# Retention, MLP and gated attention on one core: states with full height, scaling of q and k on GpSimd, low parts moved, later means in two passes

## Chip, cores and metric

One core of a Trainium2 chip runs the whole program. The metric is the device time in microseconds. PE is TensorE (matmuls and transposes), DVE VectorE, ACT ScalarE, POOL GpSimd, SP the engine that issues most DMAs.

## What is computed

Three stages follow each other, in fp32, with B = 2, 8 heads, 768 positions, head size 64 and model size 512. The first is a retention with one decay per head:

```python
for t in range(S):
    state = gamma[None, :, None, None] * state + np.einsum('bhd,bhe->bhde', k[:, :, t], v[:, :, t])
    y[:, :, t] = scale * np.einsum('bhd,bhde->bhe', q[:, :, t], state)
```

The second is a layer norm and an MLP with a residual, on the heads' outputs side by side:

```python
mu = np.mean(x, axis=-1, keepdims=True)
var = np.mean((x - mu) ** 2, axis=-1, keepdims=True)
xn = (x - mu) / np.sqrt(var + 1e-06) * g_ln
x = x + np.maximum(xn @ w_ch1, 0.0) @ w_ch2
```

The third mixes four causal attention experts by a gate that keeps the best two. The change doesn't touch it.

## The kernel before

**Retention** works on 8 pairs of heads (`it` in the code, two heads side by side in 128 columns) and 6 chunks of 128 positions, in two groups `g` of three chunks. q and k are scaled by powers of the decay (`scale_rows`, line 289: four instructions of 128x384 for a pair, k and q for each group), turned by PE (`turn`, line 596) and evicted by ACT (line 933). Then follow for a group the scores of a chunk with itself (`scores_of`, line 609), DVE's product with the causal mask (`apply_causal`, line 1149), and the chunk's own part of the output (`chunk_outputs`, line 622). What earlier chunks contribute goes through states: PE forms the outer products of k and v of five chunks (`key_values`, line 652), in PSUM bank 6, for each head 64x64, the two heads one above the other; DVE sums them up over the chunks (`states`, line 1160 copies the first, line 1165 adds the others) into `state`, a 128x128 tile for each chunk with the two heads as blocks on its diagonal and zeros elsewhere, which GpSimd has set once. PE multiplies these with the turned q (`state_outputs`, line 631), and ACT evicts the outputs to `x` (line 939).

Each engine runs its instructions in the order in which the program lists them, so the order is that of the loops over `it` at the ends of PE's and DVE's parts. PE lists pair `it + 1`'s turns, scores and outer products among pair `it`'s outputs; DVE scales pair `it + 2` between its mask products and states. SP issues the loads of pairs in the order k, q, v, three buffers deep: the k and q loads of pair n wait until pair n - 3 is scaled, its v load until the outputs of pair n - 3 are done, and the loads of the first two MLP weight tiles stand behind the last of them.

**The MLP** works in three turns of 512 positions (256 of each batch). All products are made of three passes of a shorter type (fp32r): operands are split into a high part (a rounding copy) and a low part (the rest). GpSimd splits the weights (`split_w1`, lines 492 and 494; `split_w2`); ACT writes the high parts of activations and DVE the low parts. The first turn's means come while retention still runs: DVE adds up heads (`first_sum`, line 1226), PE multiplies the sum with a 128x128 matrix of 1/512 (`first_mean`, line 639, one for each batch), DVE centres (`first_centre`, line 1232), ACT scales (line 951) and DVE writes the low part (`first_lo`, line 1238). The later two turns do the same within the turn ahead of them, by steps `f` of 16: `add_heads` at steps 9 and 10, `next_mean` (line 719, one fp32 product of 512 columns) after step 12's products, `centre` at steps 13 and 14. A step is 12 products of the first matrix (`hidden`, line 702) and 12 of the second (`project`, line 711).

## Time and profile before

| | |
|---|---|
| median of 3 runs | 482.41 us (482.4 to 483.24) |
| the profiled execution's own time | 483.22 us |
| its span | 481.5 us, granted clock 0.992 |
| busy | PE 460.7 us (96%), DVE 285.8 (59%), ACT 148.6 (31%), POOL 134.8 (28%) |
| chain that ended last | PE 84%, DVE 8%, issue 3%, ACT 3%, POOL 1% |

The span is the time from the first instruction to the last in the trace; the execution's own time includes what lies around it. The granted clock is the share of TensorE's full speed. Retention takes the first 76 us, the MLP the time to 338 us, attention the rest. A row of an order of time gives the start and the duration of one instruction, or of several alike that follow each other, and in brackets how long its engine had been idle before and what ended that.

### The profile page before, as it was taken

The page shows a single profiled execution, that of the slowest core. Times are in us where ns is not written, and L with a number is a line of the kernel's source. Part 1 is how long each engine was busy: PE and PEld are TensorE (multiplying, and loading weights), DVE is VectorE, ACT ScalarE, POOL GpSimd, SP SyncE. Part 2 cuts the span into 40 slices and gives each one's busy share as a digit, 9 for nine tenths or more (in the row PEclk, how much of TensorE's full clock was granted, in tenths as well). Part 3 has the DMA queues.
Part 4 walks back from the last instruction along what each step waited for, and adds up shares of the span by engine and source line. Part 5 has one row for each costly group of instructions (what it writes and reads, how often), then busy time and mean ns, then how long its engine had stood idle before and what let it go on. Part 6 is the DMA issues. An engine that isn't in the chain of part 4 may idle for free.

```text
span 481.5 us, 7501 instructions
## 1 busy us (share of the span) xinstructions
PE 460.7 (96%) x2762; PEld 395.5 (82%) x2762; DVE 285.8 (59%) x660; ACT 148.6 (31%) x341; POOL 134.8 (28%) x167
## 2 busy tenths in 40 slices
PE   7799979999999999999999999999999899999896
PEld 6688867888888888888788888888998799998775
DVE  3789965147633547852262886142627888888833
ACT  2334422001100311001031001131425677777833
POOL 2000007899950000000002000000501477666720
PEclk9899989999999999999999999999999999999999
DMA  7977502444400000000003000000135354343024
GB/s 172 222 173 180 141 1 66 132 131 132 131 23 0 0 0 0 0 1 0 0 13 98 0 0 1 0 1 0 23 92 129 95 124 113 88 115 83 1 100 164
DMA packets 65792, 33.04 MB, mean 69 GB/s; under 512 B 47584, under 2 KB 61920, under 8 KB 65760
## 3 DMA queue, kind: packets, MB, share of 16 engines
q1 hardware_dynamic: 64960, 32.43, 26.0%
q8 instruction: 19, 0.31, 0.3%
q10 hardware_dynamic: 800, 0.20, 0.2%
q14 instruction: 13, 0.11, 0.1%
HBM read 20.03 MB, written 3.15 MB: 48 GB/s over the span
## 4 chain that ended last, share of the span: by engine, by line
PE 84%; DVE 8%; issue 3%; ACT 3%; POOL 1%; DMA 0%; POOLq 0%; ACTq 0%; DVEq 0%
PE ps L702 27%; PE ps L711 27%; PE ps L784 5%; PE ps L835 4%; PE ps L756 3%; PE ps L803 3%; PE ps L609 3%; PE ps L818 2%; PE ps L862 2%; PE ps L622 2%; PE ps L631 2%; DVE a L1432 2%; PE ps L596 1%; DVE state L1165 1%; DVE a_low_lo L1440 1%
## 5 line engine op out<-in xcount | busy, mean ns | idle before, releaser
L1278 DVE SCALAR_TENSOR_TENSOR h_t_lo<-ps,h_t_hi 128x512 fp32r<-128x512 f32 x48 | 33.2, 692 | 126.7 <-ACT h_t_hi L988 126.7
L988 ACT ACTIVATE h_t_hi<-ps 128x512 fp32r<-128x512 f32 x48 | 28.7, 598 | 218.9 <-PE ps L702 218.9
L702 PE MATMUL ps<-xn_t_hi,w_hi 128*128 128x512 f32 x192 | 75.6, 394 | 0.7 <-DVE xn_t_lo L1238 0.7
L702 PE MATMUL ps<-xn_t_hi,w_lo 128*128 128x512 f32 x192 | 74.8, 389 | 0.0
L702 PE MATMUL ps<-xn_t_lo,w_hi 128*128 128x512 f32 x192 | 74.7, 389 | 0.0
L711 PE MATMUL ps<-w_hi,h_t_lo 128*128 128x512 f32 x192 | 74.7, 389 | 0.0
L711 PE MATMUL ps<-w_hi,h_t_hi 128*128 128x512 f32 x192 | 74.7, 389 | 0.0
L711 PE MATMUL ps<-w_lo,h_t_hi 128*128 128x512 f32 x192 | 74.7, 389 | 0.0
L554 POOL TENSOR_SCALAR a<-a,inv_den,weight 128x768 f32<-128x768 f32 (+5 forms) x48 | 34.0, 716 | 50.8 <-DVE inv_den L1452 50.4
L702 PEld LDWEIGHTS ps<-xn_t_hi,w_hi 128*128 128x128 f32 x192 | 36.1, 188 | 9.1 <-POOL w_lo L494 0.9
L702 PEld LDWEIGHTS ps<-xn_t_lo,w_hi 128*128 128x128 f32 x192 | 36.1, 188 | 7.7 <-issue 0.5
L711 PEld LDWEIGHTS ps<-w_hi,h_t_lo 128*128 128x128 f32 x192 | 36.1, 188 | 7.5
L702 PEld LDWEIGHTS ps<-xn_t_hi,w_lo 128*128 128x128 f32 x192 | 36.0, 188 | 7.5
L711 PEld LDWEIGHTS ps<-w_hi,h_t_hi 128*128 128x128 f32 x192 | 36.0, 188 | 7.5
L711 PEld LDWEIGHTS ps<-w_lo,h_t_hi 128*128 128x128 f32 x192 | 36.0, 188 | 7.5
L1040 ACT ACTIVATE a<-a,neg_max 128x768 f32<-128x768 f32 (+5 forms) x48 | 32.3, 674 | 14.5 <-DVE neg_max L1432 14.5
L1265 DVE STREAM_TRANSPOSE rows<-x 32x512 f32<-32x512 f32 x48 | 33.7, 702 | 1.4
L517 POOL TENSOR_SCALAR w_vg_hi<-raw_vg 128x1040 fp32r<-128x1040 f32 x1 | 1.1, 1064 | 118.8 <-DMA raw_wo<-in_moe_wo 118.8
L492 POOL TENSOR_SCALAR w_hi<-raw_w 128x512 fp32r<-128x512 f32 x16 | 10.8, 675 | 68.0 <-DVE head_sum L1226 66.8
L1432 DVE CUSTOM_DVE_ANT_0 a<-ps,masked 128x768 f32<-128x768 f32 (+5 forms) x48 | 27.8, 617 | 1.0 <-PE ps L803 1.0
L818 PE MATMUL ps<-ident,a 128*128 128x128 f32 x168 | 23.6, 276 | 3.5 <-DVE a_low_lo L1440 2.4
L818 PEld LDWEIGHTS ps<-ident,a 128*128 128x128 f32 x168 | 18.6, 141 | 6.6 <-POOL a L554 5.0
(140 smaller groups left out, 886.0 us busy)
## 6 DMA issues: line engine op xcount, KB each, us to landing
raw_w<-in_moe_w_ch SPq DMA_DIRECT2D x32, 256.0 KB, 2.9
k_twice_hi<-pj_hi SPq DMA_DIRECT2D x32, 96.0 KB, 2.1
k_twice_lo<-pj_lo SPq DMA_DIRECT2D x32, 96.0 KB, 2.1
out_y<-out_sb SPq DMA_DIRECT2D x12, 256.0 KB, 2.0
raw_k<-in_k SPq DMA_DIRECT2D x7, 384.0 KB, 4.3
raw_q<-in_q SPq DMA_DIRECT2D x7, 384.0 KB, 4.9
raw_v<-in_v SPq DMA_DIRECT2D x7, 384.0 KB, 3.2
q_both<-pj_hi SPq DMA_DIRECT2D x16, 96.0 KB, 2.1
```

Of the source, the lines that this page charges most:

```text
L554: pool.tensor_scalar(a[:, g % AB, c0:c1], a[:, g % AB, c0:c1], inv_den[:, u:u + 1], weight[:, u, e:e + 1], ALU.mult, ALU.mult).then_inc(s_ ...
L609: mm = pe.matmul(s_bank()[:, j, c], k_t[rows, it % 2, G * g + c, :], q_t[rows, it % 2, G * g + c, :], start=True, stop=True)
L702: mm = pe.matmul(ps[:, f % 2, :], w1[a_][:, f, kk, :], xn_t[b_][:, kk, :], start=(kk == 0 and p_ == 0), stop=(kk == KT - 1 and p_ == 2))
L711: mm = pe.matmul(ps[:, 2 + tau, :], h_t[a_][:, f % 2, tau * P:(tau + 1) * P], w2[b_][:, f, :], start=(f == 0 and p_ == 0), stop=(f == NF - ...
L784: mm = pe.matmul(pj_bank(n), w_qk[a_][n // 4 % 2][:, kk, :], x2[b_][:, b, kk, half_cols(n)], start=(kk == 0 and p_ == 0), stop=(kk == KT - ...
L818: mm = pe.transpose(flat(4, 6, s0 + P)[:, s0:s0 + P], a[:, g % AB, s0:s0 + P], ident[:, :])
L835: mm = pe.matmul(z_bank(top)[:, skip:HALF], ev[:, b * NC + sc, e].rearrange("p h d -> p (h d)"), (a_top if top else a_low)[part][:, sc, sk ...
L988: act.activation(h_t["hi"][:, f % 2, :], ps[:, f % 2, :], ACT.Relu).then_inc(s_hhi, 1)
L1040: act.activation(a[:, g % AB, c0:c1], a[:, g % AB, c0:c1], ACT.Exp, bias=neg_max[:, 2 * (g % AB) + w:2 * (g % AB) + w + 1], scale=-1.0, ac ...
L1265: dve.transpose(rows[quad(a_), :, :, :, quad(d_)].rearrange("p b k u d -> p (b k) u d"), x[quad(d_), :, U * n:U * n + U, quad(a_)]).then_i ...
L1278: dve.scalar_tensor_tensor(h_t["lo"][:, f % 2, :], ps[:, f % 2, :], 0.0, f32(h_t["hi"][:, f % 2, :]), ALU.max, ALU.subtract).then_inc(s_hl ...
L1432: dve.tensor_tensor_reduce(a[:, g % AB, c0:c1], sc_bank(g, c1)[:, c0:c1], masked[:, NC - 1 - i:NC, :].rearrange("p c t -> p (c t)"), -1.0, ...
```

## The change

There are four edits.

1. *Outer products and states.* The outer products go to blocks on the diagonal of 128x128 tiles in PSUM (five tiles of 128 columns, in bank 6 and the start of bank 7), so that their off-diagonal blocks keep the zeros that DVE writes there once at the start (a new instruction, 128x640). A state step is then one instruction of 128x128 in place of two of 64x64: five for a pair in place of ten. GpSimd's clearing of `state` goes. The first means move to other columns of bank 7. The outer products of pair 0 stand ahead of the second scores of that pair, and wait for the zeros; those of pair 6 now wait until the first centring has read bank 7.
2. *Scaling.* DVE scales pairs 0 and 1 only; GpSimd scales pairs 2 to 7, ahead of its first weight splits, whose wait for the last sum of heads is dropped.
3. *Low parts.* The four low parts of the first batch (`first_lo(0, kk)`) move from DVE's last turn of the loop to after it, behind one more sum. `first_mean(0)` moves into the next pair, behind `state_outputs`.
4. *Later means.* `next_mean` is two fp32r passes over a high and a low part of the sum in place of one fp32 product. ACT writes the high part at step 11 and DVE the low part at step 12; the product comes after step 13 and `centre` at steps 14 and 15.

Its core as a diff:

```diff
-            return ps[:, 6, 0:(NC - 1) * D].rearrange("p (c e) -> p c e", c=NC - 1)
+            return ps[:, 6:8, :].rearrange("p a n -> p (a n)")[:, 0:(NC - 1) * P].rearrange("p (c e) -> p c e", c=NC - 1)
...
-            pool.memset(state[:, :, :, :], 0.0).then_inc(s_const, 1)
...
-            pool.wait_ge(s_acc, sums_before(1))
+            def scale_pair(n):
+
+                for g in range(2):
+                    for which in "kq":
+                        if n == 2 and g == 0:
+                            pool.wait_ge(s_scaled[which], 2 * n)
+                        if n == 2 and (g, which) == (0, "k"):
+                            pool.wait_ge(s_tab_rest, 16)
+                        if n >= RB and g == 0:
+                            pool.wait_ge(s_t, 4 * (n - RB) + 4)
+                            if which == "k":
+                                pool.wait_ge(s_kv, n - RB + 1)
+                        scale_rows(pool, n, which, g)
+
+            for n in range(2, NIT):
+                scale_pair(n)
             split_w1(0)
             split_w1(1)
...
+                else:
+                    pe.wait_ge(s_zeros, 1)
+                if it == HP + 2:
+                    pe.wait_ge(s_xc, KT)
...
+            key_values(0)
             for it in range(NIT - 1):
                 scores_of(it, 1)
-                if it == 0:
-                    key_values(0)
...
                 state_outputs(it, 0)
+                if it == HP + 1:
+                    first_mean(0)
...
-                if it == HP:
-                    first_mean(0)
...
-                pe.wait_ge(s_acc, (KT - 1) * i + sums_before(2))
-                pe.matmul(mean_bank(), mean_of[:, :], head_sum[:, :], start=True, stop=True).then_inc(s_mean, 1)
+                pe.wait_ge(s_sumlo, i + 1)
+                for part in ("hi", "lo"):
+                    mm = pe.matmul(mean_bank(), mean_of[:, :], sum_part[part][:, :], start=(part == "hi"), stop=(part == "lo"))
+                mm.then_inc(s_mean, 1)
...
+                    if f == 11 and not last:
+                        act.wait_ge(s_acc, sums_before(i + 2))
+                        act.activation(sum_part["hi"][:, :], head_sum[:, :], ACT.Copy).then_inc(s_sumhi, 1)
...
-                for j in range(2):
-                    half = slice(j * D, (j + 1) * D)
-                    dve.tensor_copy(state[half, it % 2, 0, half], kv_bank()[half, 0]).then_inc(s_st, 1)
+                dve.tensor_copy(state[:, it % 2, 0], kv_bank()[:, 0]).then_inc(s_st, 1)
                 for c in range(1, NC - 1):
-                    for j in range(2):
...
+                    dve.wait_ge(s_st, (NC - 1) * it + c)
+                    dve.tensor_tensor(state[:, it % 2, c], kv_bank()[:, c], state[:, it % 2, c - 1],
+                                      ALU.add).then_inc(s_st, 1)
...
+            dve.memset(kv_bank(), 0.0).then_inc(s_zeros, 1)
...
+                    if not last and f == 12:
+                        dve.wait_ge(s_sumhi, i + 1)
+                        dve.tensor_tensor(sum_part["lo"][:, :], head_sum[:, :], f32(sum_part["hi"][:, :]),
+                                          ALU.subtract).then_inc(s_sumlo, 1)
...
-                elif it < NIT - 2:
-                    for n in "kq":
-                        scale_next(it + 2, n, 0)
-                else:
+                if it == NIT - 2:
                     states(it + 1)
...
-                if it == HP + 2:
-                    for kk in range(KT):
-                        first_lo(0, kk)
                 apply_causal(it + 1, 0)
...
-                for n in "kq":
-                    scale_next(it + 2, n, 1)
             first_sum(1, HP - 2)
+            for kk in range(KT):
+                first_lo(0, kk)
             first_sum(1, HP - 1)
```

Where the instructions moved: the first place is PE at the start, from the turns of pair 0's second group on (x6 stands for three chunks and two heads). Before, and then with the change:

```order
L596 MATMUL ps<-ident,scaled_k 128x128 x3
L596 MATMUL ps<-ident,scaled_q 128x128 x3
L609 MATMUL ps<-q_t,k_t 128x128 x6
L652 MATMUL ps<-raw_v,scaled_k 64x64 x10
L622 MATMUL ps<-prob,raw_v 64x128 x6
L631 MATMUL ps<-q_t,state 128x128 x2
```

```order
L616 MATMUL ps<-ident,scaled_k 128x128 x3
L616 MATMUL ps<-ident,scaled_q 128x128 x3
L674 MATMUL ps<-raw_v,scaled_k 64x64 x10
L629 MATMUL ps<-q_t,k_t 128x128 x6
L642 MATMUL ps<-prob,raw_v 64x128 x6
L649 MATMUL ps<-q_t,state 128x128 x2
```

The ten outer products stand ahead of the second scores now, directly behind the turns.

The second place is DVE from the states of pair 6 to the end of the loop and the mask product behind it (`prob`), before and with the change:

```order
L1160 COPY state<-ps 64x64 x2
L1165 TENSOR_TENSOR state<-ps,state 64x64 x8
L289 TENSOR_TENSOR scaled_k<-raw_k,decay_sb 128x384
L289 TENSOR_TENSOR scaled_q<-raw_q,decay_sb 128x384
L1149 TENSOR_TENSOR prob<-ps,causal 128x768
L1160 COPY state<-ps 64x64 x2
L1165 TENSOR_TENSOR state<-ps,state 64x64 x8
L1222 TENSOR_TENSOR head_sum<-x 128x256
L1238 SCALAR_TENSOR_TENSOR xn_t_lo<-centred,g_col,xn_t_hi 128x256 x4
L1149 TENSOR_TENSOR prob<-ps,causal 128x768
L1226 TENSOR_TENSOR head_sum<-head_sum,x 128x256 x2
L1149 TENSOR_TENSOR prob<-ps,causal 128x768
```

```order
L1184 COPY state<-ps 128x128
L1187 TENSOR_TENSOR state<-ps,state 128x128 x4
L1175 TENSOR_TENSOR prob<-ps,causal 128x768
L1184 COPY state<-ps 128x128
L1187 TENSOR_TENSOR state<-ps,state 128x128 x4
L1234 TENSOR_TENSOR head_sum<-x 128x256
L1175 TENSOR_TENSOR prob<-ps,causal 128x768
L1238 TENSOR_TENSOR head_sum<-head_sum,x 128x256
L1250 SCALAR_TENSOR_TENSOR xn_t_lo<-centred,g_col,xn_t_hi 128x256 x4
L1238 TENSOR_TENSOR head_sum<-head_sum,x 128x256
L1175 TENSOR_TENSOR prob<-ps,causal 128x768
```

The scaling between the mask products is gone, a pair's states are five instructions, and the four low parts stand behind the mask product of pair 7's first group, between two sums.

The third place is POOL behind its constants, with the semaphores that each instruction waits for, before and with the change:

```order
L486 AFFINE_SELECT masked<-masked 128x128 [waits s_const]
L492 TENSOR_SCALAR w_hi<-raw_w 128x512 [waits s_w1raw0,s_acc]
L494 TENSOR_TENSOR w_lo<-raw_w,w_hi 128x512 [waits s_w1hi]
L492 TENSOR_SCALAR w_hi<-raw_w 128x512 [waits s_w1raw1]
L494 TENSOR_TENSOR w_lo<-raw_w,w_hi 128x512 [waits s_w1hi]
```

```order
L491 AFFINE_SELECT masked<-masked 128x128 [waits s_const]
L295 TENSOR_TENSOR scaled_k<-raw_k,decay_sb 128x384 [waits s_load_k2,s_tab_rest,s_scaled_k]
L295 TENSOR_TENSOR scaled_q<-raw_q,decay_sb 128x384 [waits s_load_q2,s_scaled_q]
L295 TENSOR_TENSOR scaled_k<-raw_k,decay_sb 128x384 [waits s_load_k2]
L295 TENSOR_TENSOR scaled_q<-raw_q,decay_sb 128x384 [waits s_load_q2]
L295 TENSOR_TENSOR scaled_k<-raw_k,decay_sb 128x384 [waits s_load_k0,s_kv,s_t]
```

Pair 2's four instructions wait for loads and for DVE's scaling of pair 1 alone; from pair 3 on the first of a pair also waits until PE has turned the pair three before it. 19 more follow in this pattern, then the weight splits, whose first no longer waits for `s_acc`.

## Rows read from the trace of the kernel before

**Rows 1.** Stages: from:to, us, busy PE PEld DVE ACT POOL, clock, DMA, GB/s.
```profile
14.00:21.00 7.00, 6.15 (x61) 4.81 (x61) 3.99 (x8) 2.46 (x5) 0.00 (x0) 0.76 0.93 210
57.00:76.00 19.00, 14.24 (x146) 11.86 (x146) 14.10 (x38) 6.23 (x15) 3.74 (x4) 0.91 0.06 16
76.00:338.00 262.00, 262.00 (x1154) 216.00 (x1153) 129.45 (x210) 38.83 (x66) 61.09 (x62) 1.00 0.11 32
```

**Rows 2.** TensorE in order of time, from 9 us: start us, us, line, [idle before <-releaser].
```profile
9.49 0.94 PE L609 MATMUL ps<-q_t,k_t 64*128 64x128 f32 x12 [0.64 <-ACT q_t L933]
13.83 0.71 PE L631 MATMUL ps<-q_t,state 128*128 128x128 f32 x4 [2.02 <-DVE state L1165]
22.44 0.94 PE L609 MATMUL ps<-q_t,k_t 64*128 64x128 f32 x12
```

**Rows 3.** Orders of time of TensorE, VectorE and GpSimd, 60 to 76 us.
```profile
60.68 0.80 PE L652 MATMUL ps<-raw_v,scaled_k 128*64 128x64 f32 x20 [0.61 <-DVE scaled_k L289]
67.42 1.55 PE L622 MATMUL ps<-prob,raw_v 128*64 128x128 f32 x12 [2.97 <-issue]
75.53 0.47 PE L702 MATMUL ps<-xn_t_hi,w_hi 128*128 128x512 f32 x1 [0.69 <-DVE xn_t_lo L1238]
...
64.66 1.67 DVE L1238 SCALAR_TENSOR_TENSOR xn_t_lo<-centred,g_col,xn_t_hi 128x256 fp32r<-128x256 f32 x4
73.91 1.48 DVE L1238 SCALAR_TENSOR_TENSOR xn_t_lo<-centred,g_col,xn_t_hi 128x256 fp32r<-128x256 f32 x1 [0.25 <-ACT xn_t_hi L951]
...
73.84 1.26 POOL L494 TENSOR_TENSOR w_lo<-raw_w,w_hi 128x512 fp32r<-128x512 f32 x1
```

**Rows 4.** SyncE's issues in order of time; landing of raw_v (6.5 us) and of raw_q.
```profile
4.93 2.08 SPq L439 DMA_DIRECT2D raw_v<-in_v  x4
8.28 0.73 SPq L403 DMA_DIRECT2D raw_q<-in_q  x1
12.43 1.28 SPq L403 DMA_DIRECT2D raw_q<-in_q  x1
...
raw_v<-in_v SPq DMA_DIRECT2D x2, 96.0 KB, 2.3
...
DMA to landing us min/median/max: 2.2/4.7/6.5
```

**Rows 5.** VectorE in order of time, 11 to 16 us.
```profile
11.28 0.48 DVE L1160 COPY state<-ps 64x64 f32<-64x64 f32 x2 [2.12 <-PE ps L652]
13.81 0.96 DVE L1149 TENSOR_TENSOR prob<-ps,causal 128x768 f32<-128x768 f32 x1
14.68 0.55 DVE L289 TENSOR_TENSOR scaled_k<-raw_k,decay_sb 128x384 f32<-128x384 f32 x1
15.15 0.55 DVE L289 TENSOR_TENSOR scaled_q<-raw_q,decay_sb 128x384 f32<-128x384 f32 x1
```

**Rows 6.** Groups of VectorE and GpSimd by shape; line 1278: ns min/median/max, first and last start.
```profile
L1165 DVE TENSOR_TENSOR state<-ps,state 64x64 f32<-64x64 f32 x64 | 14.2, 222 | 2.0
...
L569 POOL TENSOR_TENSOR z_t_lo<-z_sum,z_t_hi 64x384 fp32r<-64x384 f32 x14 | 14.2, 1016 | 1.2
...
L1278 DVE SCALAR_TENSOR_TENSOR h_t_lo<-ps,h_t_hi x48: 691/692/693, 79.2 to 334.0; 128x512 fp32r<-128x512 f32 x48
```

**Rows 7.** TensorE in order of time, 40 to 59 us.
```profile
40.29 0.94 PE L609 MATMUL ps<-q_t,k_t 64*128 64x128 f32 x12 [0.26 <-ACT k_t L933]
51.57 0.94 PE L609 MATMUL ps<-q_t,k_t 64*128 64x128 f32 x12
58.32 0.94 PE L609 MATMUL ps<-q_t,k_t 64*128 64x128 f32 x12
```

**Rows 8.** Chain of waits, 141 to 150 us: start us, us, what.
```profile
143.85 0.86 PE ps L719 x2
144.72 2.77 PE ps L702 x12
147.48 2.72 PE ps L711 x12
```

More of the change, by code:

```diff
@@ L123, in retention_moe_program @@
             z_sum = sb(late, "z_sum", [P, 2, HALF])
+        with ExitStack() as early:
+            sum_part = {part: sb(early, f"sum_{part}", [P, N], F32R) for part in ("hi", "lo")}
         with ExitStack() as early:
@@ L268, in mean_bank, with first_mean_bank @@
             return ps[:, 7, :]
+        def first_mean_bank():
+            return ps[:, 7, P:P + U * P]
         def kv_bank():
[L271 removed]
+            return ps[:, 6:8, :].rearrange("p a n -> p (a n)")[:, 0:(NC - 1) * P].rearrange("p (c e) -> p c e", c=NC - 1)
         def part_of(g):
@@ L635, in first_mean @@
             def first_mean(b):
-                pe.wait_ge(s_const, 6)
+                pe.wait_ge(s_const, 5)
                 pe.wait_ge(s_acc, (HP - 1) * (b + 1))
-                pe.matmul(half_of(mean_bank(), b), mean_of[:, :], half_of(head_sum, b), start=True, stop=True,
+                pe.matmul(first_mean_bank(), f32(mean_of[:, :]), half_of(head_sum, b), start=True, stop=True,
                           skip_group_check=True).then_inc(s_mean, 1)
@@ L651, in key_values @@
                         rows = slice(j * D, (j + 1) * D)
-                        mm = pe.matmul(kv_bank()[rows, c], scaled["k"][:, it % RB, c, rows], raw["v"][:, it % RB, j, c],
+                        mm = pe.matmul(kv_bank()[rows, c, rows], scaled["k"][:, it % RB, c, rows], raw["v"][:, it % RB, j, c],
                                        start=True, stop=True)
@@ L727, in mlp @@
                     project(i, f - 1)
-                    if not last and f == 12:
+                    if not last and f == 13:
                         next_mean(i)
@@ L1157, in states @@
                     dve.wait_ge(s_y, y_turn(it - 2, 1) + 1)
-                for j in range(2):
-                    half = slice(j * D, (j + 1) * D)
-                    dve.tensor_copy(state[half, it % 2, 0, half], kv_bank()[half, 0]).then_inc(s_st, 1)
+                dve.tensor_copy(state[:, it % 2, 0], kv_bank()[:, 0]).then_inc(s_st, 1)
                 for c in range(1, NC - 1):
-                    for j in range(2):
-                        half = slice(j * D, (j + 1) * D)
-                        dve.wait_ge(s_st, 2 * (NC - 1) * it + 2 * c + j - 1)
-                        dve.tensor_tensor(state[half, it % 2, c, half], kv_bank()[half, c], state[half, it % 2, c - 1, half],
-                                          ALU.add).then_inc(s_st, 1)
-            def scale_next(n, which, g):
-                if n >= NIT:
-                    return
-                if n >= RB:
-                    dve.wait_ge(s_t, 4 * (n - RB) + 4)
-                    if which == "k":
-                        dve.wait_ge(s_kv, n - RB + 1)
-                scale_rows(dve, n, which, g)
+                    dve.wait_ge(s_st, (NC - 1) * it + c)
+                    dve.tensor_tensor(state[:, it % 2, c], kv_bank()[:, c], state[:, it % 2, c - 1],
+                                      ALU.add).then_inc(s_st, 1)
+            dve.memset(kv_bank(), 0.0).then_inc(s_zeros, 1)
             dve.wait_ge(s_tab, 16)
@@ L1307, in mlp @@
                             add_heads(i + 1, kk)
-                    if not last and f in (13, 14):
-                        centre(i + 1, 2 * (f - 13))
-                        centre(i + 1, 2 * (f - 13) + 1)
+                    if not last and f in (14, 15):
+                        centre(i + 1, 2 * (f - 14))
+                        centre(i + 1, 2 * (f - 14) + 1)
                     if last and f == 12:
```

23 lines of the change are left out of this document (9 added, 14 removed).

## Prediction

> **What bounds the kernel now.** I read the busy shares first: TensorE (PE) is busy 96% of the span, so a gain has to come from PE's idle time, from its clock, or from work that PE no longer does. The stage table tells where it idles: from 76 us on PE hardly waits, while in the first 76 us there are holes, and two stretches with a granted clock under 1 (full speed): a mean of 0.76 over 14 to 21 us and 0.91 over 57 to 76 us [rows 1]. The clock has two levels, 1.2 and 2.4 GHz, so these means are 3.4 us each at the lower level, and work at half speed loses half of that time, 1.7 us each. Before the first stretch PE had idled 2.02 us for the states [rows 2], before the second 2.97 us [rows 3]. I then read VectorE (DVE) in order of time against PE's waits: in the first 76 us DVE ends the long ones, directly or because what PE needs stands in DVE's queue behind other work.
>
> **Part 1, the start (states, and the outer products ahead).** PE is free at 8.85 us (9.49 less 0.64 of idle) and waits there for an eviction [rows 2]. The outer products of pair 0 move into this gap. They need the four v loads, issued in 2.08 us from 4.93 on, the last near 6.5; with 2.3 us to landing [rows 4] they are there at 8.8. So I start them at 8.85 and end them 0.80 later (a block of 20 has 0.80 in [rows 3]), at 9.65. States now take 2.53 us from 11.28 to 13.81 [rows 5]: ten instructions. Afterwards there are five of double width and height. No row shows that shape: 64 columns take 222 ns [rows 6], 384 columns 0.55 us [rows 5], so 1.03 ns for each further column and 288 ns for 128 of them; bounds are 222 and 550 ns. I take 0.29, near the narrow row, plus the 0.03 us by which the ten instructions are apart: 1.6 us, to 11.25. The mask product (0.87 to the next start, [rows 5]) ends at 12.1, and pair 1's scaling starts at 12.15 instead of 14.68. Its second instruction meets another limit: q of pair 1 is issued at 8.28 and lands a median 4.7 us later [rows 4], at 13.0, so it runs at 13.0 instead of 15.15: 2.15 us earlier, not 2.5, and PE's turns follow. The state wait of 2.02 shrinks to almost nothing and the remaining idle time is in pieces of 0.75 us or less, so I take the clock to stay at 2.4 GHz, which gives back 1.7 us. GpSimd's first pair, pair 2, waits for q of pair 2, issued at 12.43 and so there at 17.1 [rows 4]; its first q half is scaled at 18.2. PE wants it some 0.4 us ahead of its next scores (22.44 before, [rows 2], and about 18.6 after), just then; I take off 0.25 for that. **Start: 2.15 + 1.7 - 0.25 = 3.6 us.**
>
> **Part 2, scaling on GpSimd.** 24 instructions leave DVE, 4 for a pair. On GpSimd a two-input instruction with 384 elements per partition takes 1016 ns [rows 6], so a pair costs it 4.1 us. Its bounds are 0.55 (DVE's own row) and, were the broadcast operand to cost double, 2.03 us. PE's period is 6.75 us (51.57 to 58.32, a stretch without a wait, [rows 7]), so GpSimd has room up to 1.69 us for one. GpSimd idles in this stage now, and its input is early: SP issues pair n's k and q behind the v load of pair n - 1, which waits for the outputs of pair n - 4; PE turns pair n nearly two periods, 13 us, after those, and issue and landing take some 6 us of that. SP's queue keeps its order; its waits on scaled rows end no later than its wait on the outputs ahead of them. DVE keeps two mask products, five state instructions and a sum per pair: 1.74 + 1.6 + 0.35 = 3.7 us of 6.75, so the mask product comes as soon as the scores are there. Now it is late: at 40.29 PE waits 0.26 us [rows 7]; the view names an ACT copy, but the same instruction also waits on the mask product of the other half. From 22.44 to 58.32 are 35.88 us [rows 2, 7]; five periods of 6.75 and one mean product, for which I put half of the 0.86 us that twice the columns take [rows 8], make 34.18. **Middle: 1.7 us.** Moving that mean product later in the program keeps its cost; its four readers on DVE hold bank 7, for which PE's next outer products now wait, but PE has turns, scores and the outputs of half a pair to do in between.
>
> **Part 3, the end of the loop.** DVE computes the four low parts (1.67 us) from 64.66 on, ahead of the mask product of pair 7, and PE idles 2.97 us until 67.42; the outer products of pair 7 wait 0.61 us for DVE's scaling [rows 3]. Both go: the scaling is long done and the low parts move behind the mask product, into a gap in which DVE waits for an output. Next late is that mask product itself, behind states (1.6) and a sum: about 0.3 us. The half-speed stretch, 1.7 us, goes with the idle time ahead of it. Last, the 0.69 us of PE before the first hidden product [rows 3]: there one low part takes 1.48 us, where four took 1.67, and a GpSimd two-input instruction runs over the same time (73.84, 1.26 us). The change drops the wait that held GpSimd's first weight splits until this moment; they now run as soon as their load has landed, which SP issues behind the last v load, over 10 us earlier; so 0.69 goes too. **End: 2.97 + 0.61 + 1.7 + 0.69 - 0.3 = 5.7 us.** The Trainium skill's page "SBUF — State Buffer", section "Who interferes with whom", says that a DVE instruction with two SBUF inputs and a GpSimd instruction that reads SBUF exclude each other for the whole instruction, while one with a single SBUF input is free of it. The trace agrees: the low part with two SBUF inputs was held, and the 48 low parts that read PSUM took 691 to 693 ns all through GpSimd's splits [rows 6]. By the rule the loop's sums (two SBUF inputs) can be held by GpSimd's scaling, at most 1.02 us each; without the rule nothing is held. DVE's free 3 us a pair cover that either way.
>
> **Part 4, later means.** A mean product now takes 0.86 us, and the block after it 2.77 instead of 2.72 us [rows 8]: 0.91. The two passes are of the type of the hidden products, 12 in 2.72 us [rows 8], so 0.45 for two. Executed twice: **0.9 us.** The added eviction and subtraction (128x512 each, some 0.69 us as the low part of that width, [rows 6]) lie on ACT and DVE, which in this stage are busy 38.83 and 129.45 us of 262 [rows 1]. Centring moves one step later; the first normalised tile is then ready some 3 us after the last hidden product, and PE has 5.44 us of projections (24 products, twice the 2.72 of 12) until it needs it: nothing.
>
> **Sum.** 3.6 + 1.7 + 5.7 + 0.9 = 11.9 us. The profiled execution took 483.22 us, so it would take 471.3; it lies 0.8 over the median of the runs, 482.41, so the median becomes **470.5 us**.
>
> **Rivals.**
> A: *the clock still falls at the start, or loads set the pace there.* Half the 3.6 us hangs on the clock and two landings fit to within 0.1 or 0.2 us. Without the clock 1.7 us are missing, with loads or the held low part besides another 1 to 2: 472.2 to 474.5. For it speaks that by the reckoning above waits of 0.4 to 0.75 us stay close together near 12 to 15 us; against it that the long one is gone.
> B: *PE waits for GpSimd in each pair.* GpSimd's instruction is 0.47 us longer than DVE's; if all 24 were on the path, 11.2 us would come back: 481.7, the same as before. Against it: loads lie ahead by most of a period. The Trainium skill's "GPSIMD Engine Reference", section 4.1, advises against it: two-input elementwise work is to stay on VectorE, GpSimd being about half as fast. The trace agrees on the ratio (1016 ns against 0.55 us), but not that it must be paid.
> C: *slower.* GpSimd is the bound. Should the broadcast factors with three strides cost much more than the row of [rows 6], its four instructions set the period. Above 1.69 us each it costs time, above 2.2 it decides: 6 pairs x (4 x 2.2 - 6.75) = 12.3 us, all of the gain. At 2.5 us a pair takes 10: 470.5 + 19.5 = 490. Against it: the two GpSimd rows shown, 1016 ns for 384 elements and 1.26 us for 512 [rows 3, 6], agree on some 2.5 ns an element, and neither is near three times that.
>
> **How the numbers follow.** Forecast 0.66; A 0.23; B 0.03; C 0.04; better by 2 us or more (idle time I did not see as such) 0.04. The range takes the forecast with its bounds and A: 467.8 to 474.5. About 0.2%, 1 us, is what a measurement can tell here: B counts as the same with 0.02, C as slower with 0.04, the rest is faster, 0.94.
>
> **What would show it.** Right: PE's rows of scores with a period of 6.75 us and no wait above 0.3 us from the third pair on; granted clock 1.00 in all of the first 70 us; five state rows near 0.29 us a pair; GpSimd rows of 1.0 us; the first hidden product near 64.5 us (75.53 less 11.0); no low part above 0.5 us in front of it; mean products of 0.45 us. Wrong: a stretch of clock 0.5 after 12 us (A), turns that wait for GpSimd (B), GpSimd busy without a break through the loop (C), or a hidden product that waits at a step's turn, which would mean that the later centring isn't free.

## The result, and the profile after

The changed kernel takes **470.99 us** (median of 4 runs, 470.56 to 471.55) against 482.44 us before (482.4 to 483.24): a ratio of 0.9759, 95% interval 0.9743 to 0.9776. The forecast was 470.5 us, range 467.8 to 474.5. The profiled execution took 470.56 us, with a span of 468.8 us and a granted clock of 1.0.

The stages first, as in [rows 1]; retention now ends near 65 us, so the limits differ. Columns: from:to, us, busy PE PEld DVE ACT POOL, clock, DMA, GB/s.

```profile
14.00:21.00 7.00, 6.88 (x89) 5.80 (x90) 3.67 (x8) 2.73 (x6) 3.23 (x4) 1.00 1.05 238
57.00:65.00 8.00, 7.22 (x81) 5.83 (x78) 6.66 (x16) 2.73 (x6) 0.00 (x0) 1.00 0.01 2
65.00:326.00 261.00, 261.00 (x1153) 216.16 (x1152) 130.64 (x211) 39.85 (x68) 61.02 (x62) 1.00 0.12 33
```

Both stretches that had a clock of 0.76 and 0.91 have 1.00, that is 2.4 GHz all through. TensorE in order of time shows three marks that [rows 2, 3, 7] have too: the second half of pair 1's scores (18.92, was 22.44), that of pair 6's (53.09, was 58.32) and the first hidden product (64.34, was 75.53), and every wait of 0.3 us or more from 9 us to there.

```profile
9.01 0.80 PE L674 MATMUL ps<-raw_v,scaled_k 128*64 128x64 f32 x20 [0.61 <-issue]
12.83 0.55 PE L616 MATMUL ps<-ident,scaled_k 128*128 128x128 f32 x3 [0.62 <-DVE scaled_k L295]
18.92 0.94 PE L629 MATMUL ps<-q_t,k_t 64*128 64x128 f32 x12
53.09 0.94 PE L629 MATMUL ps<-q_t,k_t 64*128 64x128 f32 x12
58.68 0.88 PE L642 MATMUL ps<-prob,raw_v 128*64 128x128 f32 x12 [0.30 <-issue]
62.84 0.88 PE L642 MATMUL ps<-prob,raw_v 128*64 128x128 f32 x12 [0.48 <-issue]
64.34 0.47 PE L723 MATMUL ps<-xn_t_hi,w_hi 128*128 128x512 f32 x1
```

Between the marks lie what the prediction called start, middle and end. Of the waits of [rows 2, 3], those of 2.02, 0.61 and 0.69 us are gone, and 0.30 is left of that of 2.97.

VectorE's groups by shape up to 65 us, and after them GpSimd's (line, engine, operation, count | busy us, mean ns | idle before):

```profile
L1187 DVE TENSOR_TENSOR state<-ps,state 128x128 f32<-128x128 f32 x32 | 9.3, 291 | 1.1
L1250 DVE SCALAR_TENSOR_TENSOR xn_t_lo<-centred,g_col,xn_t_hi 128x256 fp32r<-128x256 f32 x6 | 2.6, 479 | 0.2 <-ACT xn_t_hi L974 0.2
L1184 DVE COPY state<-ps 128x128 f32<-128x128 f32 x8 | 2.3, 291 | 4.1 <-PE ps L674 4.1
...
L295 POOL TENSOR_TENSOR scaled_q<-raw_q,decay_sb 128x384 f32<-128x384 f32 x12 | 10.1, 840 | 4.5 <-DMA raw_q<-in_q 3.6 <-PE ps L616 0.9
L499 POOL TENSOR_TENSOR w_lo<-raw_w,w_hi 128x512 fp32r<-128x512 f32 x2 | 2.5, 1270 | 0.2
```

A state instruction takes 291 ns (0.29 was taken), a low part 479 ns, never 1.48 us; GpSimd's scaling takes 0.83 to 0.84 us, not the 1016 ns of the row it was priced by [rows 6]. The chain of waits answers to [rows 8]: a mean product is 0.47 us where it was 0.86.

```profile
138.11 0.47 PE ps L741 x2
138.57 2.76 PE ps L723 x12
```

### The profile page after: what moved, and what is told of

Its sections match the earlier page's. It is cut to its first block, busy times and chain, and to the rows that moved or that the text cites. A ratio compares the mean times of both kernels' runs of the same rounds, so it can differ in the third digit from the quotient of the medians.

```text
span 468.8 us, 7454 instructions
## 1 busy us (share of the span) xinstructions
PE 456.1 (97%) x2762; PEld 392.8 (84%) x2762; DVE 269.7 (58%) x599; ACT 149.9 (32%) x343; POOL 153.2 (33%) x190
## 4 chain that ended last, share of the span: by engine, by line
PE 87%; DVE 5%; ACT 2%; issue 2%; SPq 1%; DMA 1%; POOL 1%; POOLq 0%; ACTq 0%; DVEq 0%
PE ps L723 28%; PE ps L732 28%; PE ps L807 5%; PE ps L858 4%; PE ps L779 3%; PE ps L826 3%; PE ps L642 3%; PE ps L629 3%; PE ps L841 2%; PE ps L649 2%; PE ps L885 2%; PE ps L616 2%; DVE a L1439 2%; SPq L445 1%; DVE a_low_lo L1447 1%
## 5 line engine op out<-in xcount | busy, mean ns | idle before, releaser
L545 POOL TENSOR_SCALAR raw_qk<-raw_qk 128x256 f32<-128x256 f32 x4 | 1.6, 405 | 77.4 <-PE ps L732 76.7
```

## The experiments

Each kernel here is an edit of the changed one: seven take a part of the change back, two lengthen GpSimd's scaling, three go further. This table gives the three marks of each profiled execution, from TensorE's order of time, and the median of the runs. It is read by column: a difference in the first is one at the start, what the second adds to that lies in the loop, and what the third adds in the loop's end. Each ratio is to executions of the kernel before that were timed beside that kernel.

| kernel | pair 1's second scores | pair 6's | first hidden product | median us | ratio to before (95%) |
|---|---|---|---|---|---|
| before | 22.44 | 58.32 | 75.53 | 482.44 | |
| after | 18.92 | 53.09 | 64.34 | 470.99 | 0.9759 (0.9743 to 0.9776) |
| half-height states | 19.85 | 54.02 | 66.10 | 472.95 | 0.9809 (0.9774 to 0.9844) |
| scaling on VectorE | 18.68 | 52.84 | 64.65 | 470.81 | 0.9768 (0.9735 to 0.9802) |
| both of these | 21.14 | 57.66 | 70.41 | 476.82 | 0.9885 (0.9849 to 0.9921) |
| low parts in the loop | 18.83 | 52.99 | 65.50 | 472.48 | 0.9796 (0.9762 to 0.9830) |
| outer products late | 20.53 | 54.69 | 65.95 | 472.48 | 0.9785 (0.9751 to 0.9819) |
| weights wait | 19.09 | 53.25 | 64.51 | 472.03 | 0.9772 (0.9737 to 0.9807) |
| means in fp32 | 19.18 | 53.34 | 64.60 | 473.36 | 0.9825 (0.9789 to 0.9861) |
| scaling twice | 20.54 | 55.62 | 66.88 | 473.76 (one run) | |
| scaling three times | 21.60 | 74.38 | 87.19 | 493.55 (one run) | |
| loads on two queues | 18.87 | 53.04 | 64.29 | 471.21 | 0.9773 (0.9739 to 0.9807) |
| and k of pair 1 on GpSimd | 18.52 | 52.68 | 63.94 | 471.62 | 0.9782 (0.9745 to 0.9819) |
| and second spread on ACT | 18.37 | 52.53 | 63.78 | 471.00 | 0.9758 (0.9743 to 0.9773) |

Medians that differ by less than a microsecond or so are hardly told apart by the runs: two late transfers, shown in the last section, add some 0.8 to 1.4 us each to some executions of a kernel. The marks lie ahead of both. The first mark itself scatters by about 0.25 us: kernels whose start is that of the changed one have it at 18.68 to 19.18. TensorE's first scores of all begin anywhere from 6.58 to 7.58 us in these traces. Where the outer products of pair 0 stand ahead of the second scores, they begin at 8.95 to 9.36 all the same, behind v's landing or behind the scores.

**States with half height.** Each state step is two 64x64 instructions again, and GpSimd clears `state`; the rest is the changed kernel.

```diff
-dve.tensor_copy(state[:, it % 2, 0], kv_bank()[:, 0])
+for j in range(2):
+    dve.tensor_copy(state[half, it % 2, 0, half], kv_bank()[half, 0, half])
...
```

> The changed kernel with the states again in ten instructions of 64x64 for a pair, in place of five of 128x128 (GpSimd's clearing of the state tiles is back). Theory: states take 2.53 instead of 1.53 us; this lies on TensorE's path twice, at the start (0.9 us, since the scaling of pair 1 waits for it) and ahead of the mask product of pair 7 (1.0 us), and nowhere in the loop, where VectorE has over 2 us free in a pair: 472.9. Rival 1 (only the start counts): 471.9. Rival 2 (the start's clock falls again, 1.7 us more): 474.6.

It is 1.76 us at the first hidden product: 0.93 at the start, 0.83 at the end, nothing between. TensorE's order of time shows the start, where the state is waited for and behind it the scaling; the last row is from the stage table:

```profile
12.49 0.71 PE L652 MATMUL ps<-q_t,state 128*128 128x128 f32 x4 [0.99 <-DVE state L1194]
13.94 0.55 PE L617 MATMUL ps<-ident,scaled_k 128*128 128x128 f32 x3 [0.74 <-DVE scaled_k L295]
...
14.00:21.00 7.00, 6.80 (x86) 5.62 (x88) 4.49 (x15) 3.18 (x7) 3.24 (x4) 1.00 0.96 218
```

These waits stand where waits of 2.02 and 0.74 us stood before, yet the granted clock stays at 1.00 over 14 to 21 us. So the taller states don't explain the whole start.

**Scaling on VectorE.** GpSimd scales nothing; VectorE scales pair `it + 2` where it did.

```diff
-for n in range(2, NIT):
-    scale_pair(n)
...
+for n in "kq":
+    scale_next(it + 2, n, 1)
```

> The changed kernel with all scaling on VectorE again, in the places of the kernel before; GpSimd does only weights. Theory A, as the prediction has it (the moved scaling takes away the wait of 0.26 us or more in each pair, 1.7 us, and the 0.61 us before the outer products of pair 7): 473.3. Theory B (states of half the length alone give VectorE the room: 1.74 + 1.6 + 0.35 + 1.88 = 5.6 us of the period of 6.75, the mask product is no longer late, and the scaling on GpSimd is worth next to nothing by itself): 471.0 to 471.5, TensorE's period 6.75 us with no wait above 0.1 us.

The first hidden product moves by 0.31 us (0.24 sooner at the start, within the scatter, 0.56 later at the end), and the loop's part not at all (34.16 us between the first two marks, against 34.17). VectorE shows what is late, the mask product of pair 7:

```profile
56.42 1.27 DVE L1185 TENSOR_TENSOR state<-ps,state 128x128 f32<-128x128 f32 x4
57.61 0.41 DVE L1242 TENSOR_TENSOR head_sum<-x 128x256 f32<-128x256 f32 x1
57.94 0.95 DVE L1173 TENSOR_TENSOR prob<-ps,causal 128x768 f32<-128x768 f32 x1
```

It starts at 57.94, behind states and a sum, where the changed kernel, whose first mark is 0.24 later, has it at 57.62; TensorE waits 0.86 us for it instead of 0.30. The move of the scaling, for which part 2 of the prediction put 1.7 us, is worth half a microsecond at the loop's end by itself, and nothing in the middle; the median, 470.81 us, doesn't show even that.

**Both taken back.** The two edits above in one kernel.

> Both halves of the change to the loop taken back within the changed kernel: states in two half-height pieces as in the kernel before (alone +1.76 us at the first hidden product) and scaling of all pairs on VectorE (alone +0.31 us). Theory: VectorE's room in a pair is what matters, and either part gives enough of it; with neither, the loop runs at the period of before. The first hidden product moves by 1.76 + 0.31 and by the 1.71 us that the loop of before lost between the second halves of scores of pair 1 and pair 6, and its wait before the last chunk of prob is 2 us or more instead of 0.30: in sum some 4 to 5.5 us, hidden at 68.5 to 70, 475.0 to 476.5 us. Rival: the parts add up and the loop of before lost its 1.71 us to something else that stays changed (outer products block-diagonal in PSUM, low parts moved): hidden at 66.4, 473.1 us.

The parts don't add up: 1.76 + 0.31 = 2.07, and together they cost 6.07 us at the first hidden product (the loop 36.52 us instead of 34.17). The 0.25 us waits of the old loop and the low clock at the start are both there again (TensorE in order of time, then the stage table):

```profile
31.95 0.94 PE L628 MATMUL ps<-q_t,k_t 64*128 64x128 f32 x12 [0.28 <-ACT k_t L957]
39.01 0.94 PE L628 MATMUL ps<-q_t,k_t 64*128 64x128 f32 x12 [0.25 <-ACT k_t L957]
64.75 0.88 PE L641 MATMUL ps<-prob,raw_v 128*64 128x128 f32 x12 [1.38 <-issue]
...
14.00:21.00 7.00, 6.81 (x68) 5.76 (x68) 4.06 (x11) 2.37 (x6) 0.00 (x0) 0.76 0.96 217
```

The theory holds, a little above its range, and the rival falls; the wait before the last chunk is 1.38 us, though, not 2 or more. Of the 4.0 us beyond the sum, 1.53 lie at the start, where the lower clock is back, 2.35 in the loop and 0.1 at its end. Of the loop's 2.35, 0.63 come in pair 6 alone: TensorE's outer products wait 0.40 us there for the first centring, which the change put ahead of them and which the kernel before doesn't have.

For the rest, VectorE's order of time shows the reason, the first state instruction of two turns of the loop:

```profile
34.32 0.47 DVE L1187 COPY state<-ps 64x64 f32<-64x64 f32 x2 [0.39 <-PE ps L675]
41.39 0.47 DVE L1187 COPY state<-ps 64x64 f32<-64x64 f32 x2 [0.39 <-PE ps L675]
```

A turn is 7.07 us, and VectorE is idle in it once, 0.39 us, until TensorE's outer products are there; the other 6.68 it works, and TensorE waits for its mask product. The kernel before has the same turn, 7.07 us (42.66 less 35.59) with 0.38 idle. The parts in the prediction's figures agree: two mask products (1.74), ten state instructions (2.53), a sum (0.35) and four scalings (2.2, or 1.9 as they start 0.47 apart, [rows 5]) make 6.5 to 6.8 us. The work alone would just fit TensorE's period of 6.75; with the 0.39 it can't. With one part taken back VectorE has room: per turn it is idle 1.13 us with the scaling on VectorE, and 1.96 with half-height states. Either part is enough.

**Low parts in the loop.** `first_lo(0, kk)` stands ahead of the mask product of pair 7 again.

```diff
+if it == HP + 2:
+    for kk in range(KT):
+        first_lo(0, kk)
 apply_causal(it + 1, 0)
...
-for kk in range(KT):
-    first_lo(0, kk)
```

> The changed kernel (470.99 us) with one part undone: the four low parts stand in VectorE's last turn of the loop again, ahead of the mask product of pair 7. Theory (what stands ahead of that mask product on VectorE is waited for by TensorE): 1.67 us more stand there, of which 0.24 us of idle time cover a part, so TensorE's wait before the last chunk outputs grows from 0.30 to about 1.7 us; the clock stays at 1.0; 472.4 us, the first hidden product 1.4 us later than 64.34. Rival 1 (VectorE has so much room now that the low parts' place is free): 471.0. Rival 2 (the idle time brings the lower clock back, as in the kernel before): 1.4 and another 1 to 1.7, 473.8.

TensorE's wait is 1.55 us where it is 0.30, and the first hidden product is 1.16 us late:

```profile
59.84 0.88 PE L642 MATMUL ps<-prob,raw_v 128*64 128x128 f32 x12 [1.55 <-issue]
```

The 2.97 us of [rows 3] were made of several parts; this order is worth a good microsecond of them, and the clock stays up behind a wait of 1.55.

**Outer products late.** Pair 0's outer products stand behind its second scores again.

```diff
-key_values(0)
 for it in range(NIT - 1):
     scores_of(it, 1)
+    if it == 0:
+        key_values(0)
```

> The changed kernel with the outer products of pair 0 behind the second scores again. Theory: the block takes 0.73 us in TensorE's order, so the scores move up by 0.85 us (they need no load) and the states move back by 0.7 us; the states are on the path to the scaling of pair 1, so the second scores of pair 1 come 0.7 us later than 18.92, but not the first low clock: 471.7. Rival 1 (the loads of pair 1 set the pace there): 471.0 to 471.2. Rival 2 (the idle time before the state outputs brings the lower clock back): 1.5 us more, 473.2.

The start loses 1.61 us, over twice what was expected. TensorE waits 1.03 us for the states; VectorE, which in the changed kernel does them while TensorE is at the scores, is idle for 2.06 us until the outer products are there (TensorE, then VectorE).

```profile
13.29 0.71 PE L649 MATMUL ps<-q_t,state 128*128 128x128 f32 x4 [1.03 <-DVE state L1188]
...
11.64 0.29 DVE L1185 COPY state<-ps 128x128 f32<-128x128 f32 x1 [2.06 <-PE ps L674]
```

About half of the loss appears not to be the edit's. TensorE's first scores of all, in the changed kernel's execution and then in this one:

```profile
6.66 0.94 PE L629 MATMUL ps<-q_t,k_t 64*128 64x128 f32 x12 [0.58 <-ACT q_t L956]
7.54 0.94 PE L629 MATMUL ps<-q_t,k_t 64*128 64x128 f32 x12 [0.58 <-ACT q_t L957]
```

This execution begins 0.88 us later. In the changed kernel's order v's landing hides that; here nothing between these scores and the states waits for a load, so it goes through. Less the 0.88, the edit costs an estimated 0.73 us, as the theory had it.

**Weights wait.** GpSimd's first weight splits wait for the last sum of heads again.

```diff
+pool.wait_ge(s_acc, sums_before(1))
 split_w1(0)
```

> The changed kernel (470.99 us; its first hidden product at 64.34 us) with GpSimd's first weight splits waiting for the last sum of heads again, as before the change. Theory (a VectorE instruction with two SBUF inputs and a GpSimd instruction with two inputs hold each other up): the splits run again while the last low parts are written, one of them takes about 1.5 instead of 0.48 us, the first hidden product comes some 0.7 us later, at 65.0; 471.7. Rival 1 (the split's place doesn't matter, the 1.48 us of the kernel before had another cause): 64.3 and 471.0. Rival 2 (the weights themselves come too late): a wait of TensorE for the split and over 1 us.

One low part is held, and so is the split beside it (VectorE, then GpSimd, in order of time):

```profile
63.81 0.49 DVE L1251 SCALAR_TENSOR_TENSOR xn_t_lo<-centred,g_col,xn_t_hi 128x256 fp32r<-128x256 f32 x1 [0.24 <-ACT xn_t_hi L975]
64.54 1.18 DVE L1251 SCALAR_TENSOR_TENSOR xn_t_lo<-centred,g_col,xn_t_hi 128x256 fp32r<-128x256 f32 x1
...
64.09 1.35 POOL L499 TENSOR_TENSOR w_lo<-raw_w,w_hi 128x512 fp32r<-128x512 f32 x1
```

The held low part starts at 64.54, takes 0.70 us longer than its neighbours and ends 0.28 us behind the split. It is the second of its four: the first hidden product doesn't wait for it (its 0.17 us are there at the first mark already), the second group of products waits 0.33 us, and from the first hidden product to the next stage it takes 262.94 us instead of 262.30. So the price is near the expected 0.7, a little later in the program.

**Means in fp32.** `next_mean` is one fp32 product again.

```diff
-for part in ("hi", "lo"):
-    mm = pe.matmul(mean_bank(), mean_of[:, :], sum_part[part][:, :], ...)
+pe.matmul(mean_bank(), f32(mean_of[:, :]), head_sum[:, :], start=True, stop=True)
```

> The changed kernel with the later means as one fp32 product again, at step 12, without the two parts of the sum, and centring at steps 13 and 14. Theory: twice 0.40 us on TensorE's path (0.86 in place of 0.47 and the block after it 2.77 in place of 2.76): 471.8. Rival (the later centring or the added instructions cost something too, so that undoing them gives back a part): 470.99 to 471.4.

The chain has the 0.86 of before:

```profile
132.93 0.86 PE ps L740 x2
133.79 2.77 PE ps L723 x12
```

From the first hidden product to the first of the next stage's products is 263.11 us instead of 262.30: 0.81 for two means, as expected. The rest of the 2.4 us lies elsewhere in this execution: 0.26 at the start, 0.8 in a wait ahead of attention, 0.9 in the last output's landing. Why all four of its runs lie so high, one trace doesn't tell; that stays open.

**Scaling twice, and three times.** GpSimd does each scaling once, or twice, more and writes the same rows again.

```diff
+for _ in range(1):   # 2 in the second kernel
+    again.then(pool.tensor_tensor(scaled[which]..., raw[which]..., factors, ALU.mult))
 scale_rows(pool, n, which, g)
```

> The changed kernel with each of GpSimd's 24 scaling instructions executed twice in sequence (0.83 us each, so 6.8 us a pair, just the period of 6.75). Theory (GpSimd runs ahead of TensorE except for its first pair): only pair 2 is late, by 1.2 us at its second turn and 0.4 at its last, then TensorE's period is 6.75 to 6.85 us: first hidden product at 66.0, 472.6. Rival (TensorE waits for GpSimd's instruction in each pair, so that its whole length is on the path): 24 x 0.83 = 20 us more, 491.

> The changed kernel with each scaling instruction executed three times: 4 x 2.5 = 10.2 us a pair. Theory (GpSimd is the bound as soon as its four instructions take longer than 6.75 us): TensorE's period becomes 10.2 us or a little more from pair 2 on, six pairs cost some 21 us: 492. In its waits the clock may fall, which costs next to nothing while TensorE waits anyway. Rival (loads run ahead so far that a part of it is hidden): 485 or less.

Twice, pair 2 is late by 1.18 and 0.20 us, and then TensorE's period is 6.97 us instead of 6.75 (34.50, 41.47, 48.44 for the second scores of pairs 3 to 5): GpSimd works without a break, and its own turn, shown by the first of a pair's four scalings, is 6.97. Three times, GpSimd sets the period: 26.82, 37.41, 48.01, 58.61 for the first scores, 10.6 apart (GpSimd with two; TensorE with three, then GpSimd with three).

```profile
37.12 1.01 POOL L528 TENSOR_TENSOR scaled_k<-raw_k,decay_sb 128x384 f32<-128x384 f32 x1
44.09 1.01 POOL L528 TENSOR_TENSOR scaled_k<-raw_k,decay_sb 128x384 f32<-128x384 f32 x1
...
26.82 0.94 PE L638 MATMUL ps<-q_t,k_t 64*128 64x128 f32 x12
36.94 0.55 PE L625 MATMUL ps<-ident,scaled_q 128*128 128x128 f32 x3 [2.20 <-POOL scaled_q L296]
37.41 0.94 PE L638 MATMUL ps<-q_t,k_t 64*128 64x128 f32 x12
...
28.84 1.74 POOL L528 TENSOR_TENSOR scaled_q<-raw_q,decay_sb 128x384 f32<-128x384 f32 x2
39.44 1.74 POOL L528 TENSOR_TENSOR scaled_q<-raw_q,decay_sb 128x384 f32<-128x384 f32 x2
```

From 28.84 to 39.44 are 10.60 us for four scalings, TensorE's period to the hundredth. So GpSimd is the bound with 1.74 us for a scaling (6.97 / 4), by 0.2 us a pair, and with 2.65; with 0.83 it isn't. That fits the 1.69 from which rival C let it cost time. Three times took 493.55 us, 3.5 more than the 490 that C gave for 2.5 us a scaling.

**Loads on two queues.** ScalarE's queue issues the second halves of four of pair 0's loads (the second group of k and q, and v).

```diff
-for j in range(1 if (n, g) in FIRST[0:2] else 2):
+for j in range(1):
...
+for n, g in FIRST[2:]:
+    act.dma_start(raw[n][:, 0, 1, part_of(g)], ...)
```

> The second halves of pair 0's first four loads are issued from ScalarE's queue instead of behind the first halves on SyncE's; SyncE is free for the later loads that much sooner. Theory: in the changed kernel the first outer products start at 9.01 after a wait of 0.61 us for an issue whose landing is that of v, so the start is set by the pace of issues on one queue; with two queues the outer products of pair 0 start 0.6 to 0.8 us sooner, the second half of pair 1's scores at about 18.2 instead of 18.92, the first hidden product at about 63.6 instead of 64.34, and the time is 470.3 us. Rival: the transfers, not their issues, set the pace; then v lands when it did, all stays as it is, within 0.2 us, 471.0.

The 0.61 us wait of the outer products is gone, and nothing else moves: the turn of pair 1 comes at 12.96 with its wait of 0.62 for VectorE's scaled k, as it did (TensorE; the last row is VectorE's first state in the changed kernel).

```profile
7.46 0.94 PE L629 MATMUL ps<-q_t,k_t 64*128 64x128 f32 x12 [0.64 <-ACT q_t L956]
9.14 0.80 PE L674 MATMUL ps<-raw_v,scaled_k 128*64 128x64 f32 x20
12.96 0.55 PE L616 MATMUL ps<-ident,scaled_k 128*128 128x128 f32 x3 [0.62 <-DVE scaled_k L295]
...
9.85 0.29 DVE L1184 COPY state<-ps 128x128 f32<-128x128 f32 x1 [1.15 <-PE ps L674]
```

The rival's time came, but the trace doesn't decide between the two. TensorE's first scores begin at 7.46 in this execution, 0.80 us later than in the changed kernel's, so it reaches the outer products only at 9.14, when v has landed in either. With the low parts in the loop and the loads as they were, the scores begin at 7.39 and the outer products at 9.07, without a wait too. And in the changed kernel VectorE is idle 1.15 us until the outer products are there, so these are on the path, as the theory had it. The median of four runs shows no gain; what two queues are worth when TensorE begins early stays open.

**Pair 1's k on GpSimd as well,** on top of the last edit.

```diff
-for n in "kq":
-    scale_rows(dve, 1, n, g)
+scale_rows(dve, 1, "q", g)
...
+scale_rows(pool, 1, "k", g)   # for both groups, ahead of pair 2
```

> The run with loads on two queues, and pair 1's k is scaled by GpSimd while VectorE scales q alone. Theory: at the start VectorE is what TensorE waits for (the turn of pair 1 waits 0.62 us for scaled k, and VectorE runs four scalings of pair 1 between masks and states); two scalings of 0.53 us taken from it bring the second half of pair 1's scores 1.0 to 1.5 us sooner than the other run, the first hidden product to about 62.4, 469.2 us. Rival: the two engines hold each other up at their SBUF reads, as seen small (VectorE's first sum 0.59 instead of 0.41 us, GpSimd's scaling 0.96 instead of 0.83), or pair 2's loads, or GpSimd's 0.83 us per scaling against VectorE's 0.53, are next in line: no sooner than the other run, 470.3, or 0.5 later.

The marks move by 0.35 us, a third of what the theory wanted and little more than the scatter: the wait of 0.62 for k becomes one of 0.29 for q. The median doesn't show it.

**The second spread from ScalarE's queue,** on top of both: what the runs pointed to as the best version. `spread_lo` holds the last three of the six issues of a spread.

```diff
-sp.wait_ge(s_pjlo, n + 1)
...
+if n != 1:
+    spread_lo(sp, n)
...
+spread_lo(act, 1)
```

> The run with loads on two queues and pair 1's k on GpSimd (first hidden product 0.40 us sooner than in the changed kernel, but 471.62 us, its last output landing late), and the low halves of the second projection are spread from ScalarE's queue, no longer as the sixth to eighth issue in a row on SyncE. Theory: the wait of 0.7 to 1.2 us ahead of attention's first scores, which some executions show and others don't, comes from SyncE's last pair of issues before them, 1.24 us in some executions and 1.9 or more in others; with it on another queue the wait is gone in the profiled execution, values to first scores take 23.05 us or less, and the median is 0.4 us for the start and some 0.3 for the wait below the changed kernel: 470.3 us, range 469.8 to 471.0. Rival: the landing is late for another reason, or ScalarE's three issues hold up its next eviction: the stretch from values to scores is 23.7 us or more, 471.0 to 471.8.

In its trace the first hidden product is 0.56 us ahead of the changed kernel, the stretch from values to scores is 22.77 us (23.06 there), and the chain's last output transfer starts at 462.58 instead of 463.48. The last landing then takes 0.9 us longer than there, and the median is the same, 471.00. TensorE doesn't wait ahead of attention in this trace; but it doesn't in the changed kernel's either, so one trace doesn't show that the queue is the reason. The theory's time did not come, and no version here beats the changed kernel.

## Why the prediction came out right

**Start, 3.6 forecast, 3.52 measured: the mechanism right, the sizes partly by luck.** The states end at 11.4 instead of 13.8, q of pair 1 is scaled at 12.81 (13.0 forecast), and the clock stays at 1.00. TensorE's turn of this q, before and after:

```profile
15.76 0.64 PE L596 MATMUL ps<-ident,scaled_q 128*128 128x128 f32 x3
13.43 0.55 PE L616 MATMUL ps<-ident,scaled_q 128*128 128x128 f32 x3
```

It comes 2.33 us earlier where 2.15 were forecast, and up to 0.45 of that is chance: the first scores of all began at 7.11 in the execution before and at 6.66 in this one, and before the change a late beginning goes through. The 0.25 us taken off for pair 2's q was not needed: it is scaled at 17.56, and TensorE doesn't wait. From this turn to the mark it was 6.68 us and is 5.49, so the clock gave back 1.19 us and not 1.7. The errors cancel.

Which edit gives how much is now known: without the earlier outer products 1.61 us are lost (0.73 without the late beginning), without the taller states 0.93. In either case waits of 1.0 and 0.6 to 0.7 us return and the clock stays at 1.00; with half-height states and the scaling on VectorE it is 0.76 again, behind waits of 1.00 and 0.74, nearly those of half-height states alone. With the scaling three times the clock stays at 1.00 from 34 to 64 us, among waits of 2.20, and is 0.72 over 70 to 76 us, behind waits of 1.22 and 1.59. So the length of one wait doesn't tell in these runs whether the clock falls, and rival A may have been nearer than its 0.23. The kernel before itself differs: of the 30 executions of it that were timed beside the experiments, five had a granted clock of 0.999 or 1.00 and took 480.50 to 480.97 us; the other 25, at 0.987 to 0.993, took 482.27 to 483.69. The medians, 480.73 and 483.11, put the price of the lower clock at some 2.4 us, an estimate, where the forecast has 3.4 for its two stretches. That the idle time brings it on is not shown.

**Middle, 1.7 forecast, 1.71 measured, for the wrong reason.** The step that failed is the first of part 2, that the scaling's move takes the mask product's lateness away. Scaling on VectorE leaves the 34.17 us as they are; half-height states leave them too; both together bring back 2.35 us, or 1.72 without the 0.63 of pair 6. The forecast had counted VectorE's room with the change (3.7 of 6.75 us), but not with each part alone. The same holds for the 0.61 of part 3: with the scaling back on VectorE alone, that wait doesn't return. The size of GpSimd's instruction was also off, 0.83 for 1.016 us: the row that priced it writes fp32r, the scaling writes fp32, and the rows that write fp32r still take 1270 ns for 512 elements; that the type is the cause is not shown. It hid either way. The Trainium skill's "GPSIMD Engine Reference", section 3.1, has 4497 ns for a two-input instruction of 2048 fp32 elements, in proportion an estimate of 0.84 us for 384; the trace agrees.

**End, 5.7 forecast, 5.96 measured.** The 0.30 us left over in front of the chunk's products is just as forecast (58.68), the low parts are 0.48, and the clock is up. Among the causes, the order of the low parts is worth 1.26 us of the loop's end, half-height states 0.83, the weight splits 0.64 just behind it. The lower clock's share, 1.7 in the forecast, no run here takes back by itself; the traces give 1.76: from the products of the late chunk to the first hidden product, waits before them left out, it was 7.42 us (67.42 to 75.53, less 0.69) and is 5.66 (58.68 to 64.34), with the same instructions.

**Later means, 0.9 forecast, 0.81 measured** by the run that undoes them: (0.86 - 0.47) x 2, and 262.30 instead of 263.11 us. Nothing of the later centring shows: PE is busy for all 261 us of the stage.

**Sum, 11.9 forecast.** The three marks give 11.19 us and the means 0.81, 12.0 in all. The two profiled executions differ by 12.66, as that of the kernel before also waits 0.80 us ahead of attention (last section); the medians differ by 11.45.

**The rivals.** A fell: no stretch under 1.00. B fell: no turn waits for GpSimd. C's threshold fits the runs with two and three scalings, and the scaling is well below it. The Trainium skill's rule that GpSimd should not do two-input work ("GPSIMD Engine Reference", section 4.1) would have cost nothing to keep here: with the scaling on VectorE the median is 470.81 us. It would have cost some 4 us (6.07 less 1.76) had the states stayed as they were. The lock that the Trainium skill's "SBUF — State Buffer", section "Who interferes with whom", describes agrees with the weights run: 1.18 us for a low part of 0.48 beside GpSimd's two-input split. The low part at 63.81 took 0.49 although GpSimd's one-input instruction (63.39 to 64.01) still ran; no hold shows there.

## What to carry to other kernels

Add up one engine's work for one turn of the loop and the wait for its input in that turn, and compare the sum with the period of the engine that bounds: here VectorE's 6.68 us of work and 0.39 of waiting against TensorE's 6.75 explain the slow turn, and the 1.13 or 1.96 us of idle time with either part alone say that one of the two edits suffices and the second gives nothing there. To learn what one edit of several is worth, take it back alone and also with its partner. When a wait disappears and the time stays, look first whether the same engine came to that place later, as TensorE did in the run with two queues.

## What was not expected of the hardware

Two transfers vary from one execution to the next. The first stands ahead of attention: SyncE issues the low halves of k as a pair, and the pair takes 1.24 us in some executions and 1.86 to 2.44 in others. In the execution with half-height states, SyncE's issues and then TensorE:

```profile
344.71 1.24 SPq L439 DMA_DIRECT2D k_twice_lo<-pj_lo  x2
348.55 1.98 SPq L439 DMA_DIRECT2D k_twice_lo<-pj_lo  x2
...
352.20 0.47 PE L829 MATMUL ps<-k_twice_hi,q_both 128*128 128x512 f32 x1 [0.87 <-issue]
```

In the seven profiled executions in which the second pair took 1.86 us or more, the kernel before among them, TensorE waits 0.76 to 1.34 us for it; in the six others with this pair on SyncE, at 1.24, not at all or 0.34. In those six it is the pair after it that takes 1.93 to 2.48, and TensorE doesn't wait for it. The second is the last output. The time from issue to landing of the output's transfers, in the changed kernel's execution and then in that of the last run:

```profile
DMA to landing us min/median/max: 2.0/2.0/2.1
```

```profile
DMA to landing us min/median/max: 2.0/2.0/3.0
```

The longest is 3.0 with means in fp32 and 3.4 with pair 1's k on GpSimd; elsewhere it is 2.0 to 2.2. What decides either is open. Together they are larger than most effects in this study, so a difference under a microsecond was read from a mark in the trace that lies ahead of them.
